# Value products in chunks of 256 columns, and the first expert's weights split during the first eight heads

## What is computed

```python
scores = scale * np.matmul(q, k.transpose(0, 1, 3, 2))
scores = np.where(mask, scores, -1000000000.0)
attn = np.exp(scores - np.max(scores, axis=-1, keepdims=True))
attn = attn / (np.sum(attn, axis=-1, keepdims=True) + 1e-09)
return np.matmul(attn, v)
```

## Time and profile before

| | |
|---|---|
| three runs | 1014.76, 1020.16, 1021.29 us; median 1020.16 |
| profiled execution | span 1015.0 us from first to last instruction; the profile gives no other time for it |
| TensorE, VectorE, ScalarE, GpSimd busy | 865.7, 569.2, 349.7, 542.1 us |
| attention | to about 291 us |
| routing and scatter | to about 350 us, TensorE nearly idle |

### The profile page before, as it was taken

The page is one execution under the profiler, slowest core; times in us unless marked ns, Lnnn a source line. Parts: engine busy times, 40 slices in busy tenths (PEclk is TensorE's granted clock), DMA queues, the critical chain, the costliest instruction groups (busy, mean ns, idle before and its releaser), DMA issues.

```text
span 1015.0 us, 16573 instructions
## 1 busy us (share of the span) xinstructions
PE 865.7 (85%) x4669; PEld 734.4 (72%) x4670; DVE 569.2 (56%) x907; ACT 349.7 (34%) x586; POOL 542.1 (53%) x338
## 2 busy tenths in 40 slices
PE   4899999999932199999999999999493099999995
PEld 3788888888832078888878887878393078888884
DVE  6888888888851044444444444444273436665552
ACT  3878787877840121131112212020000212343210
POOL 6666665657134863364334615160362926798563
PEclk9999999999975599999999999999755589999998
DMA  7544345346643653354334525251262624566422
GB/s 162 151 122 125 88 116 142 104 109 252 254 147 142 217 188 124 124 171 159 124 124 145 176 74 171 76 175 52 85 184 84 217 80 166 193 241 209 156 103 93
DMA packets 70742, 147.83 MB, mean 146 GB/s; under 512 B 23296, under 2 KB 23296, under 8 KB 68416
## 3 DMA queue, kind: packets, MB, share of 16 engines
q1 hardware_dynamic: 38096, 60.77, 19.8%
q10 hardware_dynamic: 26624, 67.12, 19.8%
q0 software_dynamic: 6000, 19.68, 5.7%
HBM read 107.66 MB, written 39.88 MB: 145 GB/s over the span
## 4 chain that ended last, share of the span: by engine, by line
PE 72%; issue 8%; POOL 7%; DVE 5%; DMA 3%; ACT 2%; SPq 1%; ACTq 0%; POOLq 0%; DVEq 0%
PE banks L1209 15%; PE banks L1211 15%; PE banks L1210 15%; PE banks L1072 5%; PE banks L1090 4%; POOL rows_by_slot L664 3%; PE banks L1091 3%; PE banks L1224 3%; PE banks L1063 3%; PE banks L1064 3%; PE banks L1040 2%; PE banks L1102 2%; PE banks L1200 2%; DMA tokens_and_shared<-rows_by_slot 2%; POOL tokens_and_shared L278 2%
## 5 line engine op out<-in xcount | busy, mean ns | idle before, releaser
L648 POOL TENSOR_TENSOR arena<-raw_ring,arena 128x1024 fp32r<-128x1024 f32 x128 | 302.3, 2399 | 262.5 <-ACT arena L786 262.1
L786 ACT ACTIVATE arena<-raw_ring 128x1024 fp32r<-128x1024 f32 x128 | 133.2, 1058 | 460.2 <-PE banks L1211 278.0
L1209 PE MATMUL banks<-arena,split_x 128*128 x352 | 143.0, 406 | 16.1 <-DVE split_x L416 14.4
L1209 PE MATMUL banks<-arena,split_h 128*128 x352 | 142.4, 405 | 7.5 <-DVE split_h L444 5.9
L1211 PE MATMUL banks<-arena,split_x 128*128 x352 | 139.8, 397 | 0.0
L1210 PE MATMUL banks<-arena,split_x 128*128 x352 | 139.5, 396 | 0.0
L1211 PE MATMUL banks<-arena,split_h 128*128 x352 | 138.6, 394 | 0.0
L1210 PE MATMUL banks<-arena,split_h 128*128 x352 | 138.4, 393 | 0.0
L422 DVE TENSOR_SCALAR tokens_and_shared<-banks 128x512 f32<-128x512 f32 x88 | 60.8, 690 | 104.5 <-PE banks L1211 104.0
L912 DVE TENSOR_TENSOR arena<-banks,arena 128x384 fp32r<-128x384 f32 x192 | 99.0, 542 | 19.5 <-ACT arena L714 19.5
L906 DVE TENSOR_REDUCE top<-banks 128x1 f32<-128x768 f32 x96 | 91.1, 949 | 21.4 <-PE banks L1064 20.6
(11 more groups left out here) (161 smaller groups left out, 1466.9 us busy)
## 6 DMA issues: line engine op xcount, KB each, us to landing
raw_ring<-in_moe_w ACTq DMA_DIRECT2D x128, 512.0 KB, 3.4
rows_by_slot<-arena SPq DMA_DIRECT2D x8, 1024.0 KB, 6.0
raw_ring<-in_q SPq DMA_DIRECT2D x40, 192.0 KB, 3.5
raw_ring<-in_k SPq DMA_DIRECT2D x40, 192.0 KB, 4.0
tokens_and_shared<-rows_by_slot SPq DMA_DIRECT2D x30, 256.0 KB, 3.3
results_by_slot<-tokens_and_shared SPq DMA_DIRECT2D x29, 256.0 KB, 2.1
...
```

The source lines that it names most:

```text
L648: gp.tensor_tensor(arena[:, lo:lo + PIECE], ring[:, slot * PIECE:(slot + 1) * PIECE], arena[:, hi:hi + PIECE].bitcast(F32), ALU.subtract). ...
L786: act.activation(arena[:, hi:hi + PIECE], ring[:, slot * PIECE:(slot + 1) * PIECE], ACT.Copy).then_inc(w_high, 1)
L1209: pe.matmul(out_ap, left[:, 0, tile], hi, start=(b == 0), stop=False)
```

## The change

The value products of a head are made in three chunks of 256 query rows, as soon as two tiles of probabilities are split: chunk 0 in step 4 and chunk 1 in step 5 of the same head, chunk 2 in step 1 of the next, 12 products of 256 columns each, into one accumulator (`summed`, 256 columns of PSUM bank 7). ScalarE copies each chunk out behind the high parts, and the next chunk waits for that copy. The fold moves to step 3 of the next head, and `store_head` to step 4. The probabilities' parts then need two buffers of 256 rows, and everything of the attention stage fits into the arena's second block.

In the first block the first expert's weights are prepared during heads 0 to 7, one piece per head: SP loads piece m into two buffers in the token area (`load_early`), ScalarE makes its high part in step 3 of head m (`early_high`), GpSimd its low part (`early_low`, L671 of the new file). The four and four low parts around the scatter and the first expert's `high_parts` are gone, and ScalarE's later loads begin with the second expert. ScalarE's exponential for the second choice stands alone behind the logarithm.

The diff, cut to its core (renumbered semaphore counts, the arena's pieces of the later stage and VectorE's `store_all` indices are left out):

```diff
--- before.py
+++ after.py
...
         arena = sb("arena", [P, 2 * BLOCK], F32R)
-        at = [0]
+        at = [BLOCK]
         def carve(size):
...
-        p_hi = [carve(QT * S).rearrange("p (k q) -> p k q", k=QT) for _ in range(2)]
-        p_lo = [carve(QT * S).rearrange("p (k q) -> p k q", k=QT) for _ in range(2)]
+        p_hi = [carve(QT * CHUNK).rearrange("p (k q) -> p k q", k=QT) for _ in range(2)]
...
@@ -97,6 +100,7 @@
         kept = tokens_and_shared[:, 0:KEPT * WIDE].rearrange("p (t w) -> p t w", t=KEPT)[:, :, 0:DM]
         shared = tokens_and_shared[:, NT * WIDE:]
...
         oh_turned = bank(6, S // 2).bitcast(BF16)
-        side = bank(6, 1024)
-        o_sum = bank(7, QT * FOLD).rearrange("p (t d) -> p t d", t=QT)
+        summed = bank(7, CHUNK)
+        o_sum = bank(6, QT * FOLD).rearrange("p (t d) -> p t d", t=QT)
...
+
+        def chunk_place(j, t):
+
...
+            def load_early(i):
+
+                one = bass.ds(i, 1)
+                for c in range(2):
+                    need(sp, w_low, 2 * i - 1 + c)
...
+                    sp.dma_start(dst, src).then_inc(early_landed[c], 16)
...
-            with sp.Fori(1, HEADS // 2) as r:
+
+            def load_pair(r):
                 for j in range(2):
+                    load_v(2 * r + j - 1, 1 - j)
                     load_qk(2 * r + j, j)
-                    load_v(2 * r + j - 1, 1 - j)
                 blank(rows[0], TILES * DM, 4 * DM, r - 1)
+
+            load_early(0)
+            with sp.Fori(1, EARLY) as r:
+                load_pair(r)
+                load_early(r)
+            with sp.Fori(EARLY, HEADS // 2) as r:
+                load_pair(r)
...
-                need(gp, values_summed, 2 * (m - 1))
+                need(gp, values_summed, CHUNKS * (m - 1))
...
+            def early_low(i, c):
+                hi, lo = early_place(i, c)
+                gp.wait_ge(w_high, 2 * i + c + 1)
+                gp.tensor_tensor(lo, early_raw[c], hi.bitcast(F32), ALU.subtract).then_inc(w_low, 1)
+
+            split_v(0, 0, 0)
             split_qk(1, 1, 0)
-            split_v(0, 0, 0)
-            with gp.Fori(1, HEADS // 2) as r:
+            early_low(0, 0)
+            early_low(0, 1)
+            with gp.Fori(1, EARLY) as r:
+                split_v(2 * r - 1, 1, r - 1)
                 split_qk(2 * r, 0, r)
+                early_low(r, 0)
+                split_v(2 * r, 0, r)
+                split_qk(2 * r + 1, 1, r)
+                early_low(r, 1)
+            with gp.Fori(EARLY, HEADS // 2) as r:
                 split_v(2 * r - 1, 1, r - 1)
+                split_qk(2 * r, 0, r)
+                split_v(2 * r, 0, r)
                 split_qk(2 * r + 1, 1, r)
...
-                low_parts(s, 0, 0, 0, PIECES if s else PIECES // 2)
                 if s == 1:
+                    low_parts(1, 0, 0)
                     combine_gathers(gp)
...
-                if s == 0:
-                    low_parts(s, 0, 0, PIECES // 2, PIECES)
...
-            def o_copy(n, part):
-
-                act.wait_ge(values_summed, 2 * n + 1 + part)
-                if part == 0:
+            def o_copy(n, chunk):
+
+                act.wait_ge(values_summed, CHUNKS * n + chunk + 1)
+                if chunk == 0:
                     need(act, o_folded, n)
-                lo, hi = ((0, 512), (512, S))[part]
-                act.activation(o_sb[:, lo:hi], side[:, lo:hi], ACT.Copy).then_inc(o_copied, 1)
-
-            def high(g, j, t):
-
+                act.activation(o_sb[:, chunk * CHUNK:(chunk + 1) * CHUNK], summed, ACT.Copy).then_inc(o_copied, 1)
+
+            def high(g, n, j, t):
+
+                buf, at_q = chunk_place(j, t)
+                if t % 2 == 0:
+                    need(act, values_summed, CHUNKS * n + t // 2 - 1)
                 for c, (a, b) in enumerate(HALVES):
                     act.wait_ge(probs_turned, 2 * g + c + 1)
-                    act.activation(p_hi[j][:, a:b, t * P:(t + 1) * P],
+                    act.activation(p_hi[buf][:, a:b, at_q],
                                    turned_half(c).rearrange("p (k q) -> p k q", k=3), ACT.Copy).then_inc(high_ready, 1)
...
-            def pair(i, first=False, last=False):
+            def early_high(i, c):
+                hi, _ = early_place(i, c)
+                act.wait_ge(early_landed[c], 16 * i + 16)
+                act.activation(hi, early_raw[c], ACT.Copy).then_inc(w_high, 1)
...
                             need(act, inv_step, 2 * (n - 1))
                         act.activation(probs[t % 2], scores[t % 2], ACT.Exp, bias=top[:, t % 2:t % 2 + 1],
                                        accum_out=sums[:, j, t:t + 1]).then_inc(probs_ready, 1)
-                        if t == 0 and not first:
-                            o_copy(n - 2, 1)
                         if t > 0:
-                            if t == 1:
-                                need(act, values_summed, 2 * (n - 1))
-                            high(g - 1, j, t - 1)
+                            high(g - 1, n, j, t - 1)
                         elif follows:
-                            high(g - 1, 1 - j, QT - 1)
+                            high(g - 1, n - 1, 1 - j, QT - 1)
+                            o_copy(n - 1, 1)
+                        if t == 2 and follows:
+                            o_copy(n - 1, 2)
                         if t == 2 and prepares:
                             mask_rows(n + 1, 1 - j, False)
                             mask_rows(n + 1, 1 - j, True)
-                        if t == 5 and follows:
-                            o_copy(n - 1, 0)
-
-            pair(0, first=True)
-            with act.Fori(1, HEADS // 2 - 1) as i:
+                        if t == 3 and early:
+                            early_high(i, j)
+                        if t == 5:
+                            o_copy(n, 0)
+
+            pair(0, first=True, early=True)
+            with act.Fori(1, EARLY) as i:
...
@@ -981,7 +1034,9 @@
                                 choose(n + 1, 1 - j, 1)
                             if t == 1 and prepares:
                                 choose(n + 1, 1 - j, 2 + place)
-                            if t == 3 and not first and place == 2:
+                            if t == 4 and follows and place == 2:
+                                if first:
+                                    dve.wait_ge(const_ready, 23)
                                 store_all()
                         if t < QT - 1 or prepares:
...
@@ -1073,33 +1129,27 @@
                                           probs[t % 2][:, k * P:(k + 1) * P], ident[:, :])
                     mm.then_inc(probs_turned, 1)
-            def sum_values(n, j, part, prepares=False):
-
-
-                if part == 0:
-                    pe.wait_ge(low_ready, 2 * (QT * n + 4))
+            def sum_values(n, j, chunk):
+
+
+                pe.wait_ge(low_ready, 2 * (QT * n + 2 * chunk + 2))
+                if chunk == 0:
                     pe.wait_ge(v_split, 2 * (n + 1))
-                    need(pe, o_copied, 2 * n - 1)
-                    if prepares:
-                        pe.wait_ge(rows_ready, 2 * n + 6)
-                if part == 2:
-                    pe.wait_ge(low_ready, 2 * QT * (n + 1))
-                    need(pe, head_stored, n)
-                a, b = (512, S) if part == 2 else (0, 512)
-                for kb in range(QT) if part == 2 else range(*HALVES[part]):
-                    pe.matmul(side[:, a:b], v_both[j][:, kb, :], p_hi[j][:, kb, a:b], start=(kb == 0), stop=False)
-                    mm = pe.matmul(side[:, a:b], v_both[j][:, kb, :], p_lo[j][:, kb, a:b], start=False,
+                need(pe, o_copied, CHUNKS * n + chunk)
+                buf = (CHUNKS * j + chunk) % 2
+                for kb in range(QT):
+                    pe.matmul(summed, v_both[j][:, kb, :], p_hi[buf][:, kb, :], start=(kb == 0), stop=False)
+                    mm = pe.matmul(summed, v_both[j][:, kb, :], p_lo[buf][:, kb, :], start=False,
                                    stop=(kb == QT - 1))
-                if part:
-                    mm.then_inc(values_summed, 1)
-
-            def fold_output(n, h):
-
-
-                pe.wait_ge(o_copied, 2 * n + 2)
-                need(pe, head_stored, n)
+                mm.then_inc(values_summed, 1)
+
+            def fold_output(n, h, turned):
+
+
+                pe.wait_ge(o_copied, CHUNKS * (n + 1))
+                pe.wait_ge(rows_ready, 2 * turned)
                 for t in range(QT):
-                    mm = pe.matmul(bank(7, 512)[:, t * FOLD:(t + 1) * FOLD + GROUP], o_sb[:, t * P:(t + 1) * P],
+                    mm = pe.matmul(bank(6, 512)[:, t * FOLD:(t + 1) * FOLD + GROUP], o_sb[:, t * P:(t + 1) * P],
                                    fold_all[:, bass.ds(h * FOLD, FOLD + GROUP)], start=True, stop=True)
                 mm.then_inc(o_folded, 1)
...
@@ -1126,25 +1176,25 @@
                         if t == 0 and prepares:
```

(19 more changed lines are left out.)

65 lines of the change are left out of this document (41 added, 24 removed).

## The result

The changed kernel took **1140.5 us** (median of four runs, 1139.3 to 1141.5), the kernel before 1018.9 beside it on the same chip (four runs, 1014.8 to 1021.3): a ratio of **1.121**, 95% interval 1.118 to 1.125. The forecast was 1128, its range 1103 to 1144. The profiled execution's span is 1139.8 us, 124.8 longer than before. The experiments further down ran on other chips, where the same kernel before took 1034 us (e1 to e8) or 1021 us (e9, e10); the traces put that difference behind the attention (from the first expert product to the end, the changed kernel takes 662.0 us here and e1's 681.8 there), so compare ratios and the times of heads.

The account below looks back on a forecast made before the run. TensorE leads the attention, in a ring of short steps with ScalarE and VectorE; GpSimd has slack. Terms +108.3 + 11.2 - 3.4 - 7.5 = +108.6 on a span of 1015.0, plus 5.2 to the median, gave 1128 us, range 1103 to 1144.

Parts of the forecast that it names:

- The forecast case: Heads 1 to 7: GpSimd's low part waits for tile 3 and delays the next splits; +108.3 us, 80% for the forecast.
- long head: Each of heads 1 to 7, stalled on GpSimd's late splits: 30.5 us at full clock, 32.4 with the clock, against 16.57.
- The clock: TensorE restarts at 1.2 GHz after each long pause in heads 1 to 7: 2.0 us lost per head, upper end 3.5.
- Heads 8 to 14: Heads without pieces keep the single accumulator's copy waits: 1.4 us each, +11.2 for heads 8 to 15.
- tail: After the attention's last low part, fewer sums, copies, folds and stores remain: -3.4 us.
- routing: Four VectorE operations in the routing fall to 0.26 us once GpSimd is idle there: -7.5 us.
- SP's queue at nothing: SP's piece loads, queued behind the same round's loads, cost 0; uncovered, 3.4 us per head would show.
- The collision at nothing: GpSimd subtractions beside the attention's two-input VectorE work: up to 17 us possible, put at 0 because TensorE waits for GpSimd anyway.
- number 1: Rival: the stall in heads 1 to 7 is there but the clock holds at 1.00; 1114 us, 8%.
- Number 2: Rival: the clock stays at 1.2 GHz through most of each stalled head; 56 us more, 1185 us, 3%.
- Number 3: Rival: GpSimd isn't late, through a high part made before row tile 3; the copies' waits stay; 1030 us, 5%.
- Number 4: Rival, faster: GpSimd isn't late and the chunk waits hide behind TensorE's other work; about 1011 us, 4%.

Follow-up runs that it names:

- e1: The changed kernel with each GpSimd low part moved behind the splits of the next head: 1051.3 us, ratio 1.014 to the kernel before.
- e8: The changed kernel with 66 dummy TensorE transposes ahead of the next head's scores in heads 1 to 7: 1140.2 us, ratio 1.102.
- e9: e2 with low part m behind split_qk(m+2) and odd pieces' loads behind the next round's first loads: 1035.7 us, ratio 1.015.
- e10: e9 with each early low part also waiting until VectorE has finished its choice for the next head: 1008.3 us, ratio 0.988.
- e3: The changed kernel with dummy transposes in both TensorE waits of heads 1 to 7, 30 and 66 of them: 1136.1 us, ratio 1.099.
- e5: The changed kernel with the first expert's weights loaded and split as before, keeping the 256-column chunks: 1063.9 us, ratio 1.028.
- e2: e1 with ScalarE's copies of chunks 0 and 2 made ahead of the high parts: 1035.8 us, ratio 1.0005.
- e4: The kernel before, with all first-expert low parts behind the scatter and ScalarE's second exponential ahead of its high parts: ratio 0.9954, repeated 0.9939.

## Why the prediction was right, and where it was off

The forecast case came: GpSimd's low part waits for tile 3, and `split_v` and `split_qk` come late. e1 undoes that order alone and takes nearly all of the loss away. Step by step:

- **Shape of a long head.** Forecast: waits of 4 and 8 us; measured 3.70 and 6.55. From tile 3's exponential (145.57) to the next scores (161.99) 16.42 us, forecast 16.7. At full clock 30.5 was forecast; e3 gives 30.2. Seven waits for `qk_split` and none behind head 8's scores, as said. GpSimd's wait was put at 16 us and is 20.5; with the clock held, in e3, it is 16.8 at most, so the rest is the clock's.
- **The clock: the term that was mis-sized.** I took 2.0 us for each of seven heads, 14.0, from the recovery of 3.4 us in the earlier trace rows. e3 gives 24.6, which is 10.6 of the 15.8 us that the sum was short up to the first expert product. The slow stretch lasted 9.2 us behind the restart, not 3.4. In the earlier trace rows TensorE came back with 2.00 busy of 2; here it came back into the wait for the chunk copy, 3.91 busy of the first 5. e8 speaks for this as the reason: with no gap behind the short wait's restart the clock was back after 3.4 us, the length that the forecast used. For the restart behind the long wait it is not shown by itself. The end that I had set, 3.5 a head, was the measured value.
- **A misread row.** The first row, 28.82, is the scores of tile 5 of head 0, not those of tile 0 of head 1, which start at 30.56. So seven heads were put at 118.5 us before where they are 116.7, and the term was 1.8 too small. Counting six row tiles to a head would have shown it.
- **Heads 8 to 14.** Forecast 1.4 each, measured 1.76 in heads 9 to 14. The two places were the forecast's: waits of 0.91 us at the second chunk and 0.53 to 0.69 at the fold. e5 has the same in all heads and e2 takes it away. Head 8 lasts 22.2 us, +5.6: it starts at the slow clock behind the last long wait, which the forecast had put into head 7.
- **The range.** Its lower end, 1103, isn't the sum of the ends given: the head of 29.0 us has both chunk waits hidden and nothing lost to the clock (84.5 in place of 108.3), and with 1.6 in place of 11.2 for the other heads the two give 1095. The measured time lies at the other end, so this did no harm.
- **Head 0, tail, routing, behind the scatter.** +1.6, inside the 0 to 3 given; tail -3.5 by e10, where nothing else is mixed in (forecast -3.4); routing -7.5 to a tenth, confirmed by e4 and e5; the rest +0.4.
- **SP's queue at nothing.** True in the changed kernel: no load appears among its waits.
- **The collision at nothing.** In the changed kernel this was right, and for the reason given: the cluster operation took 0.35 us in all six heads read, since it ran while GpSimd stood. It was right only as long as TensorE was waiting for GpSimd. Once the order was mended the heads with a subtraction stayed 1.4 us longer than e10's in e2 and 3.1 in e9. Only the 3.1 is shown to be the collision with the low part; e2 and e10 differ in more than one thing. The Trainium skill, SBUF - State Buffer, section "Who interferes with whom", says that the two kinds of instruction exclude each other for a whole instruction; the runs agree (3.02 us beside a subtraction of 2.37 and the cast ahead of it, 0.62 on average with the subtraction kept apart). The 17 us that I had worked out from it and put aside are of the size that e9 shows, 24.

Of the rivals, e3 is number 1 made real: the clock holds, and the time falls by 24.6 us up to the first expert product, where I had said 14. Number 2 was nearer than its 3%: from 50 to 250 us the granted clock averages 0.72 where it was 1.00, so it is at 0.50 in over half of the long heads. But much of that time TensorE stands still anyway, and the cost is 3.5 us a head, not the 2.0 + 8. Number 3's time is e1's, ratio 1.014 where its 1030 stood for 1.010, though not its mechanism: the high part stayed where it was, and the splits went ahead of the low part. Number 4, the only faster one, is e10, 1.2% faster where it said 0.9. It needed the two moves that I had named, low parts that don't hold up the splits and copies that are hidden, and a third that I had not: keeping the subtraction away from VectorE's cluster choice.
